# A fused attention, MLP and expert kernel: attention of batches 1 to 3 among the chunks of the first MLP, 32x32 transposes on VectorE, and state times w_in per batch in small TensorE tiles

## The chip, the cores and the metric

The kernel runs on one core of a Trainium2 chip. The metric is the device time of one execution in microseconds. A core has TensorE (PE in the profile), VectorE (DVE), ScalarE (ACT), GpSimd (POOL) and SyncE (SP), which here only issues DMAs. Each engine works through its own instructions in the order written, and they meet in semaphores. SBUF and PSUM have 128 partitions; PSUM has 8 banks of 512 float32 for each partition.

## The reference

Three layers follow each other. Everything is float32.

```
B, H, S, Ns, D = 4, 8, 512, 32, 64
scores = x @ state.T / sqrt(D);   xread = softmax(scores) @ state      # S rows of a batch
scores2 = state @ x.T / sqrt(D);  sread = softmax(scores2) @ x         # Ns rows of a batch
X = rows of all batches, heads side by side                            # (2176, 512)
h = X @ w_in;  g = h * tanh(log1p(exp(h)));  Y = g @ w_out             # 512 -> 2048 -> 512
logits = normalised(Y) @ normalised(expert_emb).T / tau                # 8 experts
out = softmax(logits)[best] * relu(Y @ w1[best]) @ w2[best]            # 512 -> 1024 -> 512
```

scores and scores2 are the same numbers, normalised once over the 32 states and once over the 512 positions.

## The kernel before

**Precision.** The large products run in the faster format float32r: each operand is split into a high and a low part, and a product is three matmuls (high by high, high by low, low by high). WH and WL hold the two parts of weights, Ah and Al those of the attention's probabilities, gh and gl those of the activation. Products that are not split run in float32; one such matmul leaves two MATMUL records and two LDWEIGHTS records in the trace.

**Attention.** xread is never formed. Since xread @ w_in = softmax(scores) @ (state @ w_in), the first MLP multiplies the probabilities with M = state @ w_in. `M(i)` makes M for all four batches at once: 128 columns (4 batches by 32 states) stand in the array, and for a pair of heads in the two halves of the partitions two matmuls of 64 rows work on two banks (line 487). ScalarE copies M to Mst (line 799), SyncE stores it to the DRAM scratch `state_w_in` (line 300), and it comes back per batch later and is split into WH and WL.

For each batch b, TensorE turns x in 16 transposes of 128x128 (`turn`, line 458), forms the scores in four float32 matmuls of 512 columns (`score`, line 468), and turns the scores, the exponentials E2 and the probabilities P1 (lines 479, 519, 529). sread is 16 float32 matmuls of 64 columns with 128 weight columns (line 536). VectorE and ScalarE take maxima, exponentials, sums and reciprocals between them. All four batches are done before `H(0)`: the loop over b starts batch b+1's turning and scores inside batch b.

**First MLP.** There are 4 chunks (one a batch, 512 rows each) of 8 units, and a unit is 256 of the 2048 hidden columns. `H(u)` is 12 matmuls of 512 columns (line 555) into banks 0 and 1, `Y(u)` 24 of them (line 581) into banks 2 to 5. Between them stands the activation of a unit: on ScalarE a tanh, two squares, two exponentials and the copy to gh, on VectorE five operations of 128x1024 (`mish_q`, `mish_e`, `mish_r`, `mish_g`, `mish_lo`). TensorE's order is written out: H runs two units ahead of Y, and H(u) waits for `mish_q` of unit u-1, which empties banks 0 and 1. Each chunk c above 0 also carries the routing of the chunk before it (`route_t` turns a tile of Y, `route_l` makes its logits, `route_k` ranks, and `route_a` and `route_b` are the VectorE part).

**The rows of sread.** The 128 rows of all batches (named z) go through two units of 1024 hidden columns with unsplit weights (line 565), placed in chunk 3; `GT` turns their activation and `YB` multiplies it with w_out.

**The end of the MLP.** After the last Y come the first expert tile (`PA`, `TR`, `PB`) and the routing of z and of chunk 3; then VectorE builds the table of tiles (lines 1372 to 1435). Only with the table does ScalarE load the second expert tile (line 913), and the loop over the expert tiles begins.

## Time and profile before

| | |
|---|---|
| time, median of 3 runs | 750.76 us (748.86 to 751.18) |
| profiled execution | 747.9 us, of which its span 746.1 us |
| PE, DVE, ACT busy | 90%, 57%, 55% of the span |
| first H(0) | 104.8 us |
| first Y of chunks 0, 1, 2, 3 | 120.6, 195.35, 268.96, 342.64 us |
| last Y ends | 445.45 us |
| second expert tile begins | 482.43 us |

The profile is one execution. Its span goes from the first to the last instruction. The chain of waits is followed back from the last instruction to what released each step. A matmul record's time overlaps the next record's, so costs of a group are read from when the group begins and when the next piece of the chain begins.

### The profile page before, as it was taken

How to read it: one execution, taken by the hardware profiler on the slowest of the kernel's cores; microseconds unless marked ns; L12 is line 12 of the kernel's file. 1: busy time of each engine (PE TensorE's matmuls, PEld its weight loads, DVE VectorE, ACT ScalarE, POOL GpSimd, SP SyncE). 2: the span in 40 equal slices, each digit the busy share in tenths (PEclk: the TensorE clock that was granted, in tenths of full speed). 3: DMA queues.
4: the chain of work that ended last, by engine and by line, in shares of the span. 5: the costliest groups of instructions: out<-in, count | busy, mean ns of one | idle time of the engine just before them, and what ended most of it. 6: DMA issues, size and time to landing. Idle time of an engine off the chain costs nothing.

```text
span 746.1 us, 10419 instructions
## 1 busy us (share of the span) xinstructions
PE 670.1 (90%) x3124; PEld 527.8 (71%) x3125; DVE 424.4 (57%) x629; ACT 408.3 (55%) x517; POOL 51.1 (7%) x73
## 2 busy tenths in 40 slices
PE   4778767999899999999989799199999999999995
PEld 3355456888688878887766688177888888888884
DVE  1456558888758876887476654553361262154261
ACT  1334578878887887789664735052352262243260
POOL 2000000000001100200011001200000000000001
PEclk9999997999999999999999899599999999999999
DMA  9575595211001210121304210374270162145140
GB/s 207 129 188 168 172 294 184 84 58 56 29 1 58 84 29 1 71 72 57 112 16 155 71 56 16 119 240 138 71 239 29 43 207 92 42 126 184 43 156 4
DMA packets 51150, 76.52 MB, mean 103 GB/s; under 512 B 21507, under 2 KB 21507, under 8 KB 51120
## 3 DMA queue, kind: packets, MB, share of 16 engines
q1 hardware_dynamic: 44912, 61.14, 26.8%
q0 software_dynamic: 3040, 9.13, 3.2%
q10 hardware_dynamic: 3168, 5.86, 2.7%
q8 instruction: 17, 0.28, 0.2%
q14 instruction: 13, 0.11, 0.0%
HBM read 56.47 MB, written 20.55 MB: 103 GB/s over the span
## 4 chain that ended last, share of the span: by engine, by line
PE 67%; ACT 17%; DVE 8%; issue 6%; DMA 1%; SPq 0%; ACTq 0%; POOL 0%; DVEq 0%; POOLq 0%
PE PS L661 16%; PE PS L683 16%; PE PS L581 12%; PE PS L555 6%; ACT rr L854 3%; ACT WH L780 3%; ACT ww L844 3%; DVE ww L1156 2%; PE PS L468 2%; ACT gh L865 2%; ACT rr L852 2%; PE PS L670 2%; PE PS L565 2%; PE PS L536 2%; PE PS L624 2%
## 5 line engine op out<-in xcount | busy, mean ns | idle before, releaser
L581 PE MATMUL PS<-WH,gh 128*128 128x512 f32 x256 | 103.1, 403 | 4.7 <-DVE ysb L1188 4.7
L581 PE MATMUL PS<-WL,gh 128*128 128x512 f32 x256 | 101.6, 397 | 0.0
L581 PE MATMUL PS<-WH,gl 128*128 128x512 f32 x256 | 101.5, 397 | 0.0
L1246 DVE TENSOR_TENSOR WL<-raw,WH 128x1024 f32 (+1 forms) x48 | 56.8, 1221 | 31.8 <-ACT WH L917 31.8
L683 PE MATMUL PS<-WH,hh 128*128 (+1 forms) x168 | 68.5, 407 | 2.3 <-DVE hl L1256 2.3
L1151 DVE SCALAR_TENSOR_TENSOR qq<-ww,PS 128x1024 f32<-128x1024 f32 x34 | 41.5, 1220 | 44.2 <-ACT ww L846 43.9
L683 PE MATMUL PS<-WL,hh 128*128 (+1 forms) x168 | 66.0, 393 | 0.0
L683 PE MATMUL PS<-WH,hl 128*128 (+1 forms) x168 | 65.9, 393 | 0.0
L935 ACT ACTIVATE hh<-PS 128x512 fp32r<-128x512 f32 x42 | 22.8, 595 | 78.6 <-PE PS L670 76.6
L917 ACT ACTIVATE WH<-raw 128x1024 f32 (+1 forms) x48 | 48.5, 1056 | 31.1 <-issue 22.9
L858 ACT ACTIVATE ww<-ww,cst 128x1024 f32<-128x1024 f32 x34 | 39.2, 1153 | 39.8 <-DVE ww L1156 39.8
L581 PEld LDWEIGHTS PS<-WH,gh 128*128 128x128 f32 x256 | 48.8, 191 | 16.7 <-issue 5.9
L1156 DVE SCALAR_TENSOR_TENSOR ww<-ww,rr 128x1024 f32<-128x1024 f32 x34 | 41.7, 1225 | 27.9 <-ACT rr L854 27.9
L581 PEld LDWEIGHTS PS<-WH,gl 128*128 128x128 f32 x256 | 48.6, 190 | 11.6
L581 PEld LDWEIGHTS PS<-WL,gh 128*128 128x128 f32 x256 | 48.9, 191 | 11.0
L1251 DVE TENSOR_TENSOR yl<-PS,yh 128x512 fp32r<-128x512 f32 x21 | 14.5, 692 | 71.0 <-ACT yh L923 71.0
L661 PE MATMUL PS<-WH,yh 128*128 (+1 forms) x168 | 48.7, 412 | 4.5 <-issue 2.7
L929 ACT ACTIVATE hsb<-PS 128x512 f32<-128x512 f32 x42 | 24.5, 595 | 50.2 <-PE PS L661 48.9
L555 PE MATMUL PS<-Ah,WH 128*128 128x512 f32 x128 | 42.5, 414 | 8.2 <-DVE qq L1151 8.2
L844 ACT ACTIVATE ww<-PS 128x1024 f32<-128x1024 f32 x34 | 34.5, 1016 | 26.8 <-PE PS L555 17.9
L661 PE MATMUL PS<-WL,yh 128*128 (+1 forms) x168 | 46.7, 401 | 0.0
L661 PE MATMUL PS<-WH,yl 128*128 (+1 forms) x168 | 46.7, 401 | 0.0
(220 smaller groups left out, 1255.0 us busy)
## 6 DMA issues: line engine op xcount, KB each, us to landing
raw<-in_w SPq DMA_DIRECT2D x48, 512.0 KB, 4.2
raw<-in_w_in SPq DMA_DIRECT2D x16, 512.0 KB, 5.0
state_w_in<-Mst SPq DMA_DIRECT2D x64, 128.0 KB, 2.3
raw<-state_w_in SPq DMA_DIRECT2D x16, 512.0 KB, 3.6
yg<-by_expert ACTq DMA_DIRECT2D x22, 260.0 KB, 2.7
xb<-in_x SPq DMA_DIRECT2D x16, 256.0 KB, 5.6
raw<-in_w_out SPq DMA_DIRECT2D x8, 512.0 KB, 4.6
by_expert<-junk SPq DMA_DIRECT2D x1, 2080.0 KB, 10.3
```

What stands on the lines that cost most here:

```text
L555: mm = pe.matmul(PS[:, e, :], w[:, p // 2, o:o + P], a[:, c, g, :], start=(i == 0 and g == 0), stop=(i == 2 and g == HG - 1))
L581: mm = pe.matmul(PS[:, 2 + t, :], a[:, v % 2, e, t * P:t * P + P], w[:, 8 + p, e * 512:e * 512 + 512], start=(p == 0 and e == 0 and i == 0 ...
L661: mm = pe.matmul(PS[:, j, :], a[:, k, :], w[:, bass.ds(slot + k, 1), j * 512:j * 512 + 512].rearrange("p o n -> p (o n)"), start=(i == 0 a ...
L683: mm = pe.matmul(PS[:, 5, :], a[:, m, :], w[:, bass.ds(slot + (KT + m // 2), 1), (m % 2) * 512:(m % 2) * 512 + 512].rearrange("p o n -> p ...
L844: a.activation(ww[:, u % 2], PS[:, 0:2, :], ACT.Tanh, scale=0.5).then_inc(t_rdy, 1)
L858: a.activation(ww[:, u % 2], ww[:, u % 2], ACT.Square, bias=cst[:, 0:1]).then_inc(s_rdy, 1)
L917: a.activation(WH[:, bass.ds(slot + b, 1), :].rearrange("p o n -> p (o n)"), raw[:, b % NSTAGE], ACT.Copy).then_inc(w_hi, 1)
L929: a.activation(hsb[:, j * 512:j * 512 + 512], PS[:, j, :], ACT.Relu).then_inc(hs_rdy, 1)
L935: a.activation(hh[:, 4 * j:4 * j + 4, :], PS[:, 3 + j, :].rearrange("p (k m) -> p k m", k=4), ACT.Copy).then_inc(hh_rdy, 1)
L1151: v.scalar_tensor_tensor(out=qq[:, u % 2], in0=ww[:, u % 2], scalar=4.0, in1=PS[:, 0:2, :], op0=ALU.subtract, op1=ALU.mult).then_inc(q_rdy, 1)
L1156: v.scalar_tensor_tensor(out=ww[:, u % 2], in0=ww[:, u % 2], scalar=4.0, in1=rr[:], op0=ALU.add, op1=ALU.mult).then_inc(e_rdy, 1)
L1246: v.tensor_tensor(WL[:, bass.ds(slot + b, 1), :].rearrange("p o n -> p (o n)"), raw[:, b % NSTAGE], WH[:, bass.ds(slot + b, 1), :].rearran ...
```

## The change

Only batch 0's attention stands ahead of the first MLP. Batch c+1's stands inside chunk c: `score` after Y of unit 0, `M(c+1, 0..2)` before Y of units 5 to 7, `sread` after Y of unit 5, `sread_turned` after unit 6, `M(c+1, 3)` after unit 7. The VectorE part is dealt over the eight units (`turn_x`, `soft_1` to `soft_5`, `A_lo`, `sread_scale`), as is the ScalarE part.

TensorE's transposes of x, the scores, E2 and P1 are gone. VectorE transposes blocks of 32x32 instead. For that x lies in SBUF in another layout (X2, 16 DMAs a batch where there were 4), and the state is laid out block by block (S2, st32, stBD). sread is now 128 matmuls a batch, each on 32 partitions with 32 weight columns and 64 moving columns; the four j of a step use four different 32x32 tiles of the array and write four different groups of partitions of the same bank.

M is made per batch: 8 matmuls of 512 columns, each on 64 partitions with 32 weight columns, into four groups of 32 partitions of two banks. It is split from PSUM into WH and WL straight away (`M_hi`, `M_lo`), so the scratch, its 64 stores and 16 loads are gone, and w_in is read from DRAM once for each batch. M(c+1, 0) waits for `A_lo(c+1)`.

The units of z move to after units 2 and 3 of chunk 3, with matmuls into banks 6 and 7. At the end chunk 3 is routed before z, and `YB(2)`'s second half and `YB(3)` stand behind the last Y.

```diff
     SEQ = [("m", c, p) for c in range(B) for p in range(PC)]
-    SEQ.insert(3 * PC + 4, ("z", B, 0))
-    SEQ.insert(3 * PC + 7, ("z", B, 1))
+    SEQ.insert(3 * PC + 3, ("z", B, 0))
+    SEQ.insert(3 * PC + 5, ("z", B, 1))
...
+    STREAM = []
+    for what in ([(0, 0), 0, (0, 1), 1, (0, 2), 2, 3, (0, 3), 4, 5, 6, 7]
+                 + [(c, nb) for c in range(1, B) for nb in range(NB)] + ["z0", "z1", "z2", "z3"]):
+        if isinstance(what, int):
+            STREAM.append(("o", what))
+        elif isinstance(what, str):
+            STREAM += [("z", int(what[1]), 0), ("z", int(what[1]), 1)]
+        else:
+            STREAM += [("w", NB * what[0] + what[1], 0), ("w", NB * what[0] + what[1], 1)]
...
             def load_x(b):
-                for t in range(ST):
-                    sp.dma_start(xb[b][:, t].rearrange("p (h d) -> p h d", h=H),
-                                 x[b].rearrange("h (p t) d -> t p h d", t=ST)[t]).then_inc(in_x[b], 16)
...
+                if b >= 2:
+                    sp.wait_ge(sr_mm, b - 1)
+                for u in range(2):
+                    for j in range(4):
+                        for g in range(HG):
+                            sp.dma_start(X2[b % 2][u][32 * j:32 * j + 32, :, D * g:D * g + D], x_v[b, j, u, g]).then_inc(in_x[b], 16)
...
+                if r >= NSTAGE:
+                    kind, k, *_ = STREAM[r - NSTAGE]
+                    sp.wait_ge({"w": m_mm, "o": o_lo, "z": hz_mm}[kind], k + 1)
+                kind, k, *g = STREAM[r]
+                src = w_out_v[k] if kind == "o" else w_in_v[k % NB, g[0]]
...
+                pe.wait_ge(x_tr, 4 * b + 4)
+                if b > 0:
+                    pe.wait_ge(m_lo, NB * b)
                 for g in range(HG):
...
+            def M(c, nb, bank=6):
+                k = NB * c + nb
+                if k > 1:
+                    pe.wait_ge(m_lo, k - 1 if c == 0 else k)
+                if c == 0 and nb == 3:
+                    pe.wait_ge(sh_e, 2)
+                if nb == 0 and c > 0:
+                    pe.wait_ge(idx_rdy, c - 1)
+                    pe.wait_ge(a_lo, c + 1)
+                if nb == 1 and c > 0:
+                    pe.wait_ge(shn_rdy, 2 * c + 2)
+                if nb == 2 and c > 0:
+                    pe.wait_ge(sh_e, 2 * c + 2)
+                for g in range(HG):
+                    r = RING["w", k, g]
+                    pe.wait_ge(in_w[r % NSTAGE], 16 * (r // NSTAGE + 1))
+                    for kk in range(2):
+                        for h in range(2):
+                            j = 32 * (2 * kk + h)
+                            mm = pe.matmul(PS[j:j + 32, bank + g, :], stA[64 * h:64 * h + 64, 2 * g + kk, NS * c:NS * c + NS],
+                                           raw_v[64 * h:64 * h + 64, r % NSTAGE, kk, :], start=True, stop=True)
+                mm.then_inc(m_mm, 1)
...
+            def sread(b):
+                pe.wait_ge(e2d_rdy, b + 1)
+                if b > 0:
+                    pe.wait_ge(m_lo, NB * b + 1)
+                for g in range(HG):
+                    for t in range(16):
+                        for j in range(4):
+                            mm = pe.matmul(PS[32 * j:32 * j + 32, 6, D * g:D * g + D], E2D[32 * j:32 * j + 32, g, 32 * t:32 * t + 32],
+                                           X2[b % 2][t // 8][32 * j:32 * j + 32, t % 8, D * g:D * g + D],
+                                           start=(t == 0), stop=(t == 15))
+                mm.then_inc(sr_mm, 1)
+
+            def sread_turned(b):
+                pe.wait_ge(shn_rdy, 2 * b + 2)
+                if b > 0:
+                    pe.wait_ge(m_lo, NB * b + 2)
+                for g in range(HG):
+                    mm = pe.transpose(PS[0:D, 7, g * P:g * P + P], shn[:, g, :], ident[:])
+                mm.then_inc(sh_t, 1)
...
+            for v in range(B * PC):
+                c, p = v // PC, v % PC
+                if v + 2 < B * PC:
+                    H(v + 2)
...
+                if c < 3 and p >= 5:
+                    M(c + 1, p - 5)
...
+                if c < 3:
+                    if p == 0:
+                        if c == 0:
+                            M(0, 3)
+                        score(c + 1)
+                    if p == 5:
+                        sread(c + 1)
+                    if p == 6:
+                        sread_turned(c + 1)
+                    if p == 7:
+                        M(c + 1, 3)
...
+            for t in range(ST):
+                route_t(3, t)
+            for t in range(ST):
+                route_l(3, t)
+            YB(2, (2, 3))
+            YB(3, (0, 1))
+            route_k(3)
+            YB(3, (2, 3))
...
+            def M_hi(c, nb, bank=6):
+                k = NB * c + nb
                 act.wait_ge(m_mm, k + 1)
-                if k >= 4:
-                    act.wait_ge(m_out[k % 4], 64 * (k // 4))
...
+            def M_lo(c, nb, bank=6):
+                k = NB * c + nb
+                dve.wait_ge(m_hi, k + 1)
+                v.tensor_tensor(WL[:, k % NM].rearrange("p (g n) -> p g n", g=HG), PS[:, bank:bank + 2, :],
+                                WH[:, k % NM].rearrange("p (g n) -> p g n", g=HG).bitcast(F32), ALU.subtract).then_inc(m_lo, 1)
...
+            def turn_x(b, c):
+                dve.wait_ge(in_x[b], 256)
+                if b > 0:
+                    dve.wait_ge(sr_mm, b)
+                for u in range(2):
+                    ins = v.transpose(xT[:, c, u * 256:u * 256 + 256].rearrange("p (t n) -> p t n", n=32),
+                                      X2[b % 2][u][:, :, 32 * c:32 * c + 32])
+                ins.then_inc(x_tr, 1)
...
+            def soft_1(b):
+                dve.wait_ge(sc_e, b + 1)
+                v.transpose(PT[:], SC[:]).then_inc(av, 1)
+                dve.wait_ge(av, AV * b + 1)
+                v.tensor_reduce(r1[:, 0, :], pv, AX, ALU.max).then_inc(av, 1)
+                dve.wait_ge(av, AV * b + 2)
+                v.tensor_tensor(pv, pv, r1[:, 0, :].unsqueeze(2).to_broadcast(wide), ALU.subtract).then_inc(p1_d, 1)
...
+            def soft_4(b):
+                dve.wait_ge(pn_rdy, b + 1)
+                dve.wait_ge(s2_x, 2 * b + 2)
+                v.transpose(SC[:], PT[:]).then_inc(af_rdy, 1)
+
+            def soft_5(b):
+                dve.wait_ge(s2_x, 2 * b + 2)
+                v.tensor_scalar(r2[:, 2, :], r2[:, 2, :], 1e-9, None, ALU.add).then_inc(bv, 1)
+                dve.wait_ge(bv, 2 * b + 1)
+                v.reciprocal(r2[:, 3, :], r2[:, 2, :]).then_inc(bv, 1)
+                v.transpose(E2D[:], E2[:]).then_inc(e2d_rdy, 1)
+
+            def A_lo(b):
+                dve.wait_ge(a_hi, b + 1)
+                v.tensor_tensor(Al[:, b % 2], SC[:], Ah[:, b % 2].bitcast(F32), ALU.subtract).then_inc(a_lo, 1)
...
+                    if n == 0:
+                        turn_x(c + 1, 0)
+                        turn_x(c + 1, 1)
+                    if n == 1:
+                        turn_x(c + 1, 2)
+                        turn_x(c + 1, 3)
+                    if n == 3:
+                        soft_1(c + 1)
+                    if n == 4:
+                        soft_3(c + 1)
+                    if n == 5:
+                        soft_4(c + 1)
+                    if n == 6:
+                        A_lo(c + 1)
+                        soft_5(c + 1)
+                    if n == 7:
```

TensorE, from its first matmul on. Before (SN is the state, xb x, E and P the exponentials and probabilities):

```order
L458 MATMUL PS<-ident,xb_92 128x128 x16
L495 MATMUL PS<-ident,SN_85 128x128 x4
L468 MATMUL PS<-ysb,stT 128x512 x4
L501 MATMUL PS<-ident,E_90 128x8 x4
L479 MATMUL PS<-ident,SC 128x128 x8
L458 MATMUL PS<-ident,xb_93 128x128 x16
L468 MATMUL PS<-ysb,stT 128x512 x4
L487 MATMUL PS<-raw,stA 128x512 x4
L519 MATMUL PS<-ident,E_90 128x128 x8
L487 MATMUL PS<-raw,stA 128x512 x4
L529 MATMUL PS<-ident,P_89 128x128 x8
L536 MATMUL PS<-E_90,xb_92 128x64 x16
```

After (x_0a and x_0b are the halves of X2, E2D the turned exponentials, shn the scaled sread, WH and Ah the operands of H(0)):

```order
L494 MATMUL PS<-ident,SN_91 128x128 x4
L444 MATMUL PS<-xT,stBD 128x512 x4
L467 MATMUL PS<-raw,stA 32x512 x8
L502 MATMUL PS<-ident,en 128x8 x4
L467 MATMUL PS<-raw,stA 32x512 x8
L478 MATMUL PS<-x_0a,E2D 32x64 x32
L478 MATMUL PS<-x_0b,E2D 32x64 x32
L478 MATMUL PS<-x_0a,E2D 32x64 x32
L478 MATMUL PS<-x_0b,E2D 32x64 x32
L467 MATMUL PS<-raw,stA 32x512 x8
L488 MATMUL PS<-ident,shn 64x128 x2
L526 MATMUL PS<-Ah,WH 128x512 x2
```

Of the attention that was repeated for each batch, one batch is left ahead of the first row that reads Ah; the rows of 8 and 16 transposes are gone (three small ones are left, of the state, the expert embedding and shn), and sread has become 4 rows of 32.

VectorE, unit 6 of chunk 0 with the row ahead of it. Before (WL<-raw is the rest of a weight block):

```order
L1065 TENSOR_TENSOR WL<-raw,WH 128x1024
L1151 SCALAR_TENSOR_TENSOR qq<-ww,PS 128x1024
L1174 TENSOR_TENSOR gl<-qq,gh 128x1024
L1156 SCALAR_TENSOR_TENSOR ww<-ww,rr 128x1024
L1161 SCALAR_TENSOR_TENSOR qq<-qq,rr 128x1024
L1168 SCALAR_TENSOR_TENSOR qq<-ww,qq 128x1024
L1065 TENSOR_TENSOR WL<-raw,WH 128x1024
```

After, from the end of unit 5 on (E_53 is E2, r_68 its sums, Al<-SC is `A_lo(1)`):

```order
L1202 SCALAR_TENSOR_TENSOR qq<-ww,qq 128x1024
L1090 TENSOR_TENSOR WL<-raw,WH 128x1024
L1131 STREAM_TRANSPOSE SC<-PT 128x1024
L1185 SCALAR_TENSOR_TENSOR qq<-ww,PS 128x1024
L1208 TENSOR_TENSOR gl<-qq,gh 128x1024
L1190 SCALAR_TENSOR_TENSOR ww<-ww,rr 128x1024
L1195 SCALAR_TENSOR_TENSOR qq<-qq,rr 128x1024
L1202 SCALAR_TENSOR_TENSOR qq<-ww,qq 128x1024
L1142 TENSOR_TENSOR Al<-SC,Ah 128x1024
L1135 TENSOR_SCALAR r_68<-r_68 128x2
L1137 RECIPROCAL r_68<-r_68 128x2
L1138 STREAM_TRANSPOSE E2D<-E_53 128x1024
```

`soft_4` now follows unit 5, and `A_lo(1)` and `soft_5` unit 6; in TensorE's order M(1, 0), which waits for `A_lo(1)`, stands between H(7) and Y(5).

## Rows read from the trace of the kernel before

**Rows 1.** The page: span, busy time of the engines, the chain by engine.

```profile
span 746.1 us, 10419 instructions
PE 670.1 (90%) x3124; PEld 527.8 (71%) x3125; DVE 424.4 (57%) x629; ACT 408.3 (55%) x517; POOL 51.1 (7%) x73
...
PE 67%; ACT 17%; DVE 8%; issue 6%; DMA 1%; SPq 0%; ACTq 0%; POOL 0%; DVEq 0%; POOLq 0%
```

**Rows 2.** Stretches: length, each engine's busy us, TensorE clock, DMA share, GB/s.

```profile
0.00:104.80 104.80, 76.37 (x393) 48.17 (x394) 49.42 (x82) 43.44 (x72) 5.15 (x25) 0.97 0.70 181
104.80:120.60 15.80, 7.60 (x27) 5.47 (x26) 11.87 (x11) 14.12 (x16) 0.00 (x0) 0.85 0.86 316
120.60:195.35 74.75, 72.26 (x300) 58.22 (x301) 62.53 (x55) 63.08 (x63) 0.00 (x0) 0.96 0.21 72
195.35:268.96 73.61, 72.50 (x340) 59.70 (x341) 56.65 (x71) 59.31 (x67) 6.57 (x10) 1.00 0.13 44
...
342.64:445.45 102.81, 94.94 (x405) 72.49 (x406) 63.65 (x90) 63.49 (x74) 7.31 (x6) 0.95 0.24 80
445.45:482.43 36.98, 21.22 (x128) 17.71 (x128) 19.30 (x93) 11.45 (x23) 6.13 (x6) 0.80 0.14 48
```

**Rows 3.** The chain of waits, ahead of H(0): start, us, what.

```profile
14.52 6.57 PE PS L468 x8
...
44.48 0.88 PE PS L479 x8
...
66.18 0.88 PE PS L479 x8
```

**Rows 4.** The chain of waits in the first MLP and at its end.

```profile
201.60 2.74 PE PS L555 x12
204.34 0.79 PE PS L624 x8
205.62 5.58 PE PS L581 x24
...
359.79 6.87 PE PS L565 x16
...
389.44 8.58 PE PS L565 x16
...
404.05 2.72 PE PS L601 x12
...
467.58 0.17 DVE idx L1242
...
475.41 0.18 DVE tab L1435
```

**Rows 5.** SyncE in order of time: start, us, operation.

```profile
0.78 2.96 SPq L288 DMA_DIRECT2D xb<-in_x  x4
...
3.78 2.63 SPq L325 DMA_DIRECT2D SN<-in_state  x4
```

**Rows 6.** Groups of instructions up to 104.8 us: shapes, count | busy, mean ns | idle before.

```profile
L1071 DVE COPY ysb<-PS 128x512 f32<-128x512 f32 x8 | 5.5, 687 | 16.8 <-PE PS L458 16.8
L1136 DVE TENSOR_TENSOR P<-P,lg 128x1024 f32<-128x1024 f32 x4 | 4.9, 1224 | 0.1
...
L799 ACT ACTIVATE Mst<-PS 128x1024 f32<-128x1024 f32 x16 | 16.4, 1028 | 25.8 <-PE PS L487 25.7
```

**Rows 7.** TensorE's small products in order of time: start, us, engine, operation.

```profile
21.02 0.33 PEld L501 LDWEIGHTS PS<-ident,E 8*128 8x128 f32 x4 [0.89 <-issue]
27.44 3.67 PE L468 MATMUL PS<-ysb,stT 128*128 128x512 f32 x8 [1.12 <-ACT ysb L786]
31.04 1.13 PE L487 MATMUL PS<-raw,stA 64*128 64x512 f32 x4
40.73 3.76 PE L536 MATMUL PS<-E,xb 128*128 128x64 f32 x32
```

More of the change, by code:

```diff
@@ new lines, in H, with HB @@
+                mm.then_inc(h_mm, 1)
+            def HB(p):
+                pe.wait_ge(sh_e, 2 * B)
+                pe.wait_ge(m_lo, NB * B)
+                if p == 1:
+                    pe.wait_ge(q_rdy, Z0 + 1)
+                for e in range(2):
+                    for g in range(HG):
+                        r = RING["z", 2 * p + e, g]
+                        pe.wait_ge(in_w[r % NSTAGE], 16 * (r // NSTAGE + 1))
+                        for j in range(2):
+                            mm = pe.matmul(PS[:, 6 + e, :], sh[:, 2 * g + j, :], raw_v[:, r % NSTAGE, j, :],
+                                           start=(g == 0 and j == 0), stop=(g == 1 and j == 1))
+                    mm.then_inc(hz_mm, 1)
@@ new lines, in _ @@
+                if kind == "m" and c < 3:
+                    if n == 2:
+                        scores_out(c + 1)
+                    if n == 4:
+                        exp_2(c + 1)
+                if kind == "m" and c > 0 and n == 0:
+                    sread_out(c)
+            mish_hi(LAST)
+            load(t0)
+            whi(0, 0, 0)
+            whi(0, 1, 0)
+            split_gz(2)
+            whi(0, 2, 0)
+            split_gz(3)
+            y_hi(t0)
+            whi(0, 3, 0)
@@ new lines, in _ @@
+            pn_rdy, bv = sem("pn_rdy"), sem("bv")
+            dve.wait_ge(in_state, 192)
+            v.transpose(st32[:].rearrange("p b c n -> p (b c n)"), S2[:].rearrange("p b g d -> p (b g d)")).then_inc(st_32, 1)
+            dve.wait_ge(st_zero, 1)
+            dve.wait_ge(st_32, 1)
+            for j in range(4):
+                v.tensor_copy(stBD[32 * j:32 * j + 32, :, :, 32 * j:32 * j + 32], st32[32 * j:32 * j + 32]).then_inc(st_d, 1)
+            for c in range(2 * HG):
+                turn_x(0, c)
@@ L1142, in _ @@
-            split_lo(("m", 0, 0))
-            split_lo(("o", 0))
-            split_lo(("m", 0, 1))
-            split_lo(("o", 1))
+            v.tensor_scalar(en[:], eb[:], es[:, 2:3], None, ALU.mult).then_inc(en_rdy, 1)
+            soft_1(0)
+            soft_2(0)
+            M_lo(0, 0, 2)
+            soft_3(0)
+            soft_4(0)
+            soft_5(0)
+            dve.wait_ge(en_t, 1)
+            v.tensor_copy(enT[:], PS[:, 1, 0:KT * E].rearrange("p (k e) -> p k e", k=KT)).then_inc(enT_rdy, 1)
@@ L1149, in mish_q @@
+            A_lo(0)
+            o_rest(0)
+            M_lo(0, 1, 4)
+            sread_scale(0)
+            M_lo(0, 2, 2)
+            o_rest(1)
             def mish_q(u):
+                bank = 0 if SEQ[u][0] == "m" else 6
                 dve.wait_ge(w_rdy, u + 1)
-                v.scalar_tensor_tensor(out=qq[:, u % 2], in0=ww[:, u % 2], scalar=4.0, in1=PS[:, 0:2, :],
+                v.scalar_tensor_tensor(out=qq[:, u % 2], in0=ww[:, u % 2], scalar=4.0, in1=PS[:, bank:bank + 2, :],
                                        op0=ALU.subtract, op1=ALU.mult).then_inc(q_rdy, 1)
@@ L1312, in _ @@
                     mish_lo(u - 1)
-                if u == Z0 + 2:
-                    lo_gz(0)
-                if u == Z0 + 3:
-                    lo_gz(1)
-                if u == LAST:
-                    lo_gz(2)
+                if kind == "m" and n < 3 and c > 0:
+                    M_lo(c, n + 1)
+                if n == 7 and c < 3:
+                    M_lo(c + 1, 0)
+                if n == 4 and c < 3:
+                    soft_2(c + 1)
+                if done >= 0 and n == (6 if c == 3 else 5):
+                    route_a(done)
@@ L1355, in _ @@
+                if c == 3 and n == 6:
+                    lo_gz(0)
+                if c == 3 and n == 7:
+                    first_expert()
+                    lo_gz(1)
+            mish_lo(LAST)
+            wlo(0, 0, 0)
+            wlo(0, 1, 0)
+            lo_gz(2)
+            wlo(0, 2, 0)
+            lo_gz(3)
+            y_lo(t0)
+            wlo(0, 3, 0)
+            y_out(3)
+            turned(3, 1)
+            turned(3, 3)
+            route_a(3)
+            route_b(3)
             y_out("z")
@@ L1363, in _ @@
             route_b("z")
-            wlo(0, 7, 0)
-            route_a(3)
-            route_b(3)
             def wide(ap):
```

807 lines of the change are left out of this document (329 added, 478 removed).

## The prediction

> **What bounds the kernel now.** I read the page first. TensorE is busy for 90% of the span and makes 67% of the chain that ended last, so the question of every edit is what it does to TensorE's work and to its idle time [rows 1]. Then I cut the execution at the first H(0), at the first Y of each chunk and at the second expert tile [rows 2]. The reader is to see three kinds of stretch there. Up to H(0) TensorE is busy for 76.4 of 104.8 us. In chunk 1 it is busy for 72.5 of 73.6 us, while DVE has 57 and ACT 59: TensorE alone sets this pace, and every microsecond put on it comes out at the end. At the end of the MLP (445.45 to 482.43) it is busy for 21 of 37 us, and what counts is the chain of routing and table. The chain of waits says what a batch costs ahead of H(0): the same row stands at 44.48 and at 66.18, so a batch takes 21.7 us [rows 3].
>
> So the change takes three batches out of a stretch in which TensorE was idle for a quarter, and puts them into one in which it was idle for 1.5%. The gain must come from the new form costing TensorE less than 21.7 us a batch. I sum on TensorE.
>
> **The prices of the new work on TensorE.** score(b) has the same shape: 3.67 us [rows 7], I take 3.7.
>
> M: two float32 matmuls of 64 rows on the two halves of the partitions take 1.13 us, four records (line 487), where eight records of the full height take 3.67, 0.43 of 512 columns each beside the last one's end [rows 7]. Alone four would take 1.7, so different halves of the rows do run together. A call of M now has 8 matmuls on four small tiles, in two rounds. If the quarters of the columns run together as the halves of the rows do, it is 2 x 1.08 = 2.2 us, at least 2.0. If only the rows do, 4 x 0.86 + 0.3 = 3.7. If nothing does, 8 x 0.86 = 6.9. I take 2.2, since the trace shows side by side work of tiles, and 14 calls are on TensorE's path: M(0,2) ahead of H(0), M(0,3), and 12 more.
>
> sread: 128 matmuls or 256 records of 64 columns a batch, where 32 records took 3.76 us, 0.117 each [rows 7]. Bounds: if the four tiles run together, one tile has 64 records at 0.43 x 64/512 = 0.054 us, 3.5 us. At the old spacing it is 256 x 0.112 = 28.7. The closest small records are four weight loads in 0.33 us of about 0.14 each, 0.064 apart (line 501), 16.4 us. Those four load 128 columns and the new ones 32, so it should be less. I take 10 us, half way between 3.5 and 16.4.
>
> The rows bound this only widely. The Trainium skill (TensorE: Matmul & The Clock Gate, "Wait — 56ns, not 53.3ns?") states a floor of about 25 ns from start to start of small matmuls, and 62 ns where the instructions are decoded in microcode. By the one an sread is 6.4 us (estimate, 256 x 25 ns) and the sum falls by 4 x 3.6 = 14 us; by the other it is 15.9 and the sum rises by 24. No row here is short enough to tell them apart.
>
> **Ahead of H(0).** Only batch 0 is left, but its loads come later. x is now 16 DMAs, then 8 of S2 and 4 of SN2. Four loads of SN took 2.63 us and four of xb 2.96 [rows 5], so 28 issues of 0.6 us would end at 18 us; with some at 0.45 and 3 us to land I take 18 for the last state. Before, TensorE began its scores at 14.5 [rows 3]. Then in one chain: on DVE st32 0.7, four copies 1.8, eight `turn_x` 2.3 (a 128x512 copy is 0.69 [rows 6]; I price a 32x32 transpose as a copy of its size); score(0) 6.6, as the first one took before at the low clock [rows 3]; scores to SBUF 1.1; `soft_1` 3.65, three operations of 128x1024 at 1.22 [rows 6]; `soft_2` 1.4; M_lo 1.2, which stands in between; `soft_3` 3.1; `soft_4` 1.2; `soft_5` 1.6; sread(0) 10; M(0,2) and the turn of sread 2.5. This gives 55.3 us for H(0), against 104.8: 49.5 us less. The start of the pipeline up to Y(0), 15.8 us with TensorE half idle [rows 2], stays.
>
> **Inside chunks 0 to 2.** Each gets 3.7 (score) + 10 (sread) + 4 x 2.2 (M) + 0.3 = 22.8 us of TensorE, and chunk 0 also M(0,3), 2.2: 70.6 us in all. That the scratch with its 64 stores and 16 loads goes saves nothing here, since no step of the chain in the MLP waits for it; the DMAs move 44 GB/s in chunk 1 [rows 2], and w_in read three times more (12 MB over some 290 us) adds 41.
>
> DVE gets 14.8 us a batch more: three transposes of 1024 and four of 512, four passes over the probabilities, one reduction, `A_lo`. 56.7 + 14.8 = 71.5 stands beside 73.6 + 22.8 = 96 of TensorE, so DVE isn't the bound of a chunk. But it is late at one place. M(c+1,0) waits for `A_lo(c+1)`, which is queued behind all of unit 6, and unit 6 behind `soft_1` to `soft_4`, which make units 3 and 4 about 10 us of DVE each where TensorE's slots are 9. Laying the units one after the other with rows of 1.22 on DVE and 1.03 on ACT [rows 6], `A_lo` ends 2.6 us after H(7), with Y(5) queued behind M: 2.6 x 3 = 7.8 us.
>
> The small tiles are light work. The second unit of z took 8.58 us where the first took 6.87 [rows 4], since the clock had fallen to the low level for a while: 1.7 us each time. I put this down once a chunk, 5.1 us. With 0 and 13 as its ends this and the wait are in the range.
>
> **Chunk 3 and the end.** Unchanged in amount: units of 2.74 + 5.58 us and some more, z's units 6.87, YB 2.72, a tile's logits 0.79 [rows 4]. It has 94.2 us of TensorE, of which the halves of YB that now stand behind the last Y (5.5 us) are no part; with 3 us of waits 97, where it took 102.8 [rows 2]. Behind the last Y the new chain is: copy out, four turns and logits, `route_a` (8.2 us), YB and rank and `route_b` (12.3), then z, whose expert work is in between (24.7), the table 7.7 (32.4; before, from 467.7 to 475.4 [rows 4]), load and turn of the next tile 7.0 (39.4; before, from 475.4 to 482.4). That is 39.4 where 37.0 were. Both together: 3 us less. It could be 8 less or 3 more.
>
> **Sum.** -49.5 + 70.6 + 7.8 + 5.1 - 3 = +31 us. The profiled execution has 746.1 of span in 747.9 of time and lies 0.4% under the median of the runs, 750.76. I add to the median: 782 us.
>
> **Rivals.**
> 1. *The small tiles run side by side almost fully.* For it: the 1.13 us of line 487. Against: nothing shows that records can be issued every 20 ns. With sread 5 and M 2.0: -54.7 + 53 + 7.8 - 3 = +3, 754 us.
> 2. *Issue or the column quarters bind.* For it: the 0.064 of line 501. sread 16.4 alone gives +57 and M 3.7 alone +52, so about 805 us; both 828.
> 3. *Tiles that write the same bank take turns.* Before, the two row halves of line 487 wrote two banks (6 and 7); now two halves, and in sread four quarters, write one bank. So the row's overlap was only seen with separate banks. M would be 6.9 and sread 28.7: -26 + 188 + 10 = +172, 922 us. The Trainium skill (TensorEngine Tiling (Array Packing), "Gotcha 1: PSUM Pressure") says just this, that different row tiles cannot access the same PSUM bank at the same time. The tiles here also write different partitions, which the rule doesn't speak of, and I give it 3 in 100.
> 4. *The prologue's gain outweighs the rest.* One mechanism: sread at its tile limit. It decides in four places, one ahead of H(0) and three in the chunks, and the sum is -52.7 + 4 x sread + 14 x M + waits and clock. With M 2.2 and 7.8 of waits it crosses zero at sread = 3.5 us. At sread 3.5, M 2.0 and 3 us of waits it is -7.7: 743 us, faster.
> 5. *DVE's transposes cost twice a copy.* Nothing in the trace shows one. Then H(0) is 6.3 us later and each chunk waits some 3 us more: 797 us.
>
> **How the numbers follow.** Forecast 0.45 (own range 765 to 800), rival 1 0.20, rival 2 0.15, rival 3 0.03, rival 4 0.12, rival 5 0.05. The likeliest time is 782. For 8 in 10 the range runs from 746 to 815: it leaves out about half of rival 4, rival 3 and the end of rival 2. Within 0.3% (2.3 us, about what can be told from no change) lies a part of rival 1, 0.04; faster is rival 4 and a little of rival 1, 0.14; slower 0.82.
>
> **What would show it.** H(0) at 55 us, with the last state DMA at 18. An L478 group of 128 matmuls 10 us long, an L467 group of 8 about 2.2. Chunks 1 and 2 some 100 us long instead of 73.6, with TensorE busy above 95%. A wait of L467 for `A_lo` (L1142) of 2 to 3 us, three times. 39 us from the last Y to the second expert tile. I am wrong if sread is under 5 or above 16 us, if M is above 3, or if TensorE waits for DVE for more than 8 us in a chunk.

## The result

The changed kernel takes 766.22 us (median of 4 runs, 763.33 to 770.77); the kernel before, run beside it, 749.81 us (745.24 to 751.18). The ratio is 1.0235, 95% interval 1.0167 to 1.0303: slower. The profiled execution took 765.84 us, of which 763.7 is the span, against 747.9 and 746.1 before.

### The profile page after: what moved, and what is told of

Its sections match the earlier page's. It is cut to its first block, busy times and chain, and to the rows that moved or that the text cites. A ratio compares the mean times of both kernels' runs of the same rounds, so it can differ in the third digit from the quotient of the medians.

```text
span 763.7 us, 12248 instructions
## 1 busy us (share of the span) xinstructions
PE 672.9 (88%) x4060; PEld 513.7 (67%) x4061; DVE 438.4 (57%) x656; ACT 385.7 (51%) x483; POOL 53.2 (7%) x73
## 4 chain that ended last, share of the span: by engine, by line
PE 58%; DVE 18%; issue 12%; ACT 7%; DMA 3%; SPq 2%; ACTq 0%; POOL 0%; DVEq 0%; POOLq 0%
PE PS L649 15%; PE PS L671 14%; PE PS L555 8%; PE PS L526 6%; PE PS L467 3%; PE PS L444 3%; DVE ww L1190 2%; PE PS L658 2%; ACT ww L870 2%; DVE qq L1202 2%; DVE qq L1185 2%; PE PS L478 2%; DVE gl L1208 1%; DMA raw<-in_w 1%; PE PS L630 1%
## 5 line engine op out<-in xcount | busy, mean ns | idle before, releaser
L555 PE MATMUL PS<-WH,gh 128*128 128x512 f32 x256 | 104.1, 407 | 0.0
L555 PE MATMUL PS<-WL,gh 128*128 128x512 f32 x256 | 101.6, 397 | 0.0
L555 PE MATMUL PS<-WH,gl 128*128 128x512 f32 x256 | 101.4, 396 | 0.0
L1185 DVE SCALAR_TENSOR_TENSOR qq<-ww,PS 128x1024 f32<-128x1024 f32 x34 | 41.2, 1211 | 65.5 <-ACT ww L858 65.5
L671 PE MATMUL PS<-WH,hh 128*128 (+1 forms) x168 | 68.7, 409 | 4.8 <-DVE hl L1294 4.8
L671 PE MATMUL PS<-WH,hl 128*128 (+1 forms) x168 | 66.9, 398 | 0.0
L671 PE MATMUL PS<-WL,hh 128*128 (+1 forms) x168 | 66.6, 397 | 0.0
L555 PEld LDWEIGHTS PS<-WH,gh 128*128 128x128 f32 x256 | 48.9, 191 | 18.8 <-issue 8.3
L555 PEld LDWEIGHTS PS<-WH,gl 128*128 128x128 f32 x256 | 48.6, 190 | 11.5
L555 PEld LDWEIGHTS PS<-WL,gh 128*128 128x128 f32 x256 | 48.9, 191 | 10.6
L526 PE MATMUL PS<-Ah,WH 128*128 128x512 f32 x128 | 45.7, 439 | 11.1 <-DVE qq L1185 11.1
L1190 DVE SCALAR_TENSOR_TENSOR ww<-ww,rr 128x1024 f32<-128x1024 f32 x34 | 41.6, 1224 | 18.7 <-ACT rr L866 18.7
```

Source lines behind the costliest of these rows:

```text
L526: mm = pe.matmul(PS[:, e, :], w[:, (NB * c + p // 2) % NM, o:o + P], a[:, c % 2, g, :], start=(i == 0 and g == 0), stop=(i == 2 and g == H ...
L555: mm = pe.matmul(PS[:, 2 + t, :], a[:, v % 2, e, t * P:t * P + P], w[:, 8 + p, e * 512:e * 512 + 512], start=(p == 0 and e == 0 and i == 0 ...
L671: mm = pe.matmul(PS[:, 5, :], a[:, m, :], w[:, bass.ds(slot + (KT + m // 2), 1), (m % 2) * 512:(m % 2) * 512 + 512].rearrange("p o n -> p ...
L1185: v.scalar_tensor_tensor(out=qq[:, u % 2], in0=ww[:, u % 2], scalar=4.0, in1=PS[:, bank:bank + 2, :], op0=ALU.subtract, op1=ALU.mult).then ...
L1190: v.scalar_tensor_tensor(out=ww[:, u % 2], in0=ww[:, u % 2], scalar=4.0, in1=rr[:], op0=ALU.add, op1=ALU.mult).then_inc(e_rdy, 1)
```

## The profile after

The page of the changed kernel, which answers to [rows 1]. TensorE is busy for about as long as before (672.9 us for 670.1), and the span is 17.6 us longer: what was added is mostly idle time of TensorE and time at the low clock.

```profile
span 763.7 us, 12248 instructions
PE 672.9 (88%) x4060; PEld 513.7 (67%) x4061; DVE 438.4 (57%) x656; ACT 385.7 (51%) x483; POOL 53.2 (7%) x73
...
PE 58%; DVE 18%; issue 12%; ACT 7%; DMA 3%; SPq 2%; ACTq 0%; POOL 0%; DVEq 0%; POOLq 0%
```

The stretches of the changed kernel, columns as in [rows 2], cut at H(0), H(2), the first Y of chunks 1, 2 and 3, the end of the last Y and the second expert tile:

```profile
0.00:50.20 50.20, 19.86 (x322) 9.77 (x324) 21.45 (x37) 10.05 (x16) 5.13 (x25) 0.90 0.44 129
50.20:65.00 14.80, 7.60 (x26) 5.48 (x24) 10.79 (x13) 12.35 (x14) 0.00 (x0) 0.86 0.76 197
65.00:172.66 107.66, 95.71 (x646) 67.84 (x647) 78.73 (x83) 66.87 (x70) 0.00 (x0) 0.92 0.39 108
172.66:267.49 94.83, 90.24 (x672) 67.04 (x670) 70.96 (x95) 64.10 (x75) 7.09 (x9) 0.98 0.17 57
267.49:360.78 93.29, 88.67 (x671) 66.36 (x670) 68.31 (x87) 64.14 (x75) 6.21 (x5) 1.00 0.18 57
360.78:455.09 94.31, 88.38 (x382) 66.59 (x381) 60.49 (x86) 61.49 (x70) 5.54 (x6) 0.98 0.25 89
455.09:499.88 44.79, 29.98 (x154) 24.44 (x152) 23.23 (x98) 13.24 (x26) 8.82 (x7) 0.82 0.12 40
```

One correction to the text ahead: what it calls the first Y of chunk 0, at 120.6 us, is H(2); Y(0) stands some 5 us behind it. The stretch is cut at H(2) in both kernels here, so the comparison holds.

| stretch | before | after | difference | forecast |
|---|---|---|---|---|
| to H(0) | 104.8 | 50.2 | -54.6 | -49.5 |
| to H(2) | 15.8 | 14.8 | -1.0 | 0 |
| chunk 0 | 74.75 | 107.66 | +32.9 | +29.3 |
| chunk 1 | 73.61 | 94.83 | +21.2 | +27.1 |
| chunk 2 | 73.68 | 93.29 | +19.6 | +27.1 |
| chunk 3 | 102.81 | 94.31 | -8.5 | -5.8 |
| end, to the second tile | 36.98 | 44.79 | +7.8 | +2.4 |
| experts | 263.67 | 263.82 | +0.2 | 0 |
| sum | 746.1 | 763.7 | +17.6 | +31 |

What TensorE waited for in the changed kernel (engine, line, releaser: us in total, times, longest):

```profile
PE PS L526 <- DVE qq L1185: 11.1, 4, 3.7
...
PE PS L467 <- DVE Al L1142: 9.0, 3, 3.0
PE PS L478 <- DVE E2D L1138: 5.2, 1, 5.2
...
PE PS L467 <- DMA raw<-in_w_in: 4.7, 3, 2.8
...
PE PS L444 <- DVE WL L1085: 4.2, 3, 3.7
PE PS L478 <- issue: 4.1, 3, 1.4
```

The two disputed prices, from the chain of waits of the changed kernel, around Y(5) of chunk 0 (L555) (start, us, what):

```profile
133.76 1.92 PE PS L467 x16
135.68 5.78 PE PS L555 x24
141.46 3.69 PE PS L478 x250
145.15 1.36 issue
146.51 0.31 PE PS L478 x6
146.82 2.96 PE PS L526 x12
```

A call of M is 8 float32 matmuls in 16 records and takes 1.9 us. An sread is 256 records in 3.7 us of work, 14 ns from start to start, and a gap of 1.4 us that no semaphore explains: 5.2 us together, where I had put 10. The gap stands behind record 250 in chunk 0, 212 in chunk 1 and 174 in chunk 2. TensorE's rows behind the first two, in order of time (x6 and x44 are the records left, in brackets the idle time ahead and what ended it):

```profile
146.51 0.31 PE L478 MATMUL PS<-x_1b,E2D 32*32 32x64 f32 x6 [1.36 <-issue]
240.80 0.86 PE L478 MATMUL PS<-x_0b,E2D 32*32 32x64 f32 x44 [1.35 <-issue]
```

Ahead of H(0), chain of the changed kernel. The last load of state lands at 16.03, and once sread is done, TensorE still waits for a block of w_in that SP, held by the ring of four buffers, could only ask for at 43.07. sread(0), from 40.84 to 46.09, isn't on the chain that ends at H(0); VectorE's work on a block of w_out (L1090), SP's request and the load run past it, and TensorE waits 1.05 and 0.84 us for w_in in M(0, 2):

```profile
21.52 6.22 PE PS L444 x8
...
41.82 1.23 DVE WL L1090
43.07 0.37 SPq L312
...
43.48 5.53 DMA raw<-in_w_in
...
49.05 1.06 PE PS L467 x8
```

In chunk 0, score(1) stands behind Y(0) and M(0, 3) and waits for the first `M_lo(0, 3)` (L1085), which on DVE is queued behind all of unit 1; the granted clock over it is 0.54, so mostly at its low level (1.2 GHz), and it takes 6.73 us and not the 3.67 of chunk 1. H(3) follows, and the mish units after it:

```profile
80.64 1.14 DVE WL L1085
81.79 0.14 issue
81.92 6.73 PE PS L444 x8
88.65 2.79 PE PS L526 x12
```

At the end, z's last ranking (L622, L623) stands behind PB (L671), the second product of the first expert tile. Chain of the changed kernel:

```profile
474.96 0.80 PE PS L614 x8
...
478.24 1.21 DVE hl L1294 x2
479.49 4.57 PE PS L671 x12
484.06 0.16 PE PS L622 x2
```

The logits of z were there at 475.76. Some 1.4 us of small VectorE operations lie between logits and ranking (so in a version below), so the table waits for a ranking that could have run some 7 us earlier. The kernel before ranks z ahead of PB: it is the change that moved it behind PB's first half.

## The experiments

Intervals are of the ratio to the kernel before, which was run beside each of three groups of versions: 752.02 us beside the first four below, 751.14 beside the next four, 750.61 beside the last three.

### The changed kernel again

> The changed kernel as it is, beside the others of this call, so that they can be compared on one chip. The theory that adds up the stretches of its profile (prologue -54.6, start of the pipeline -1.0, chunks 0 to 2 +32.9, +21.2, +19.6, chunk 3 -8.5, the end +7.8 us) expects 17 to 18 us over the kernel before, a ratio of 1.023. If that profile was a lucky or unlucky execution, the ratio will lie outside 1.017 to 1.030.

766.22 us, ratio 1.0212 (1.0169 to 1.0255), span 762.5. It is the base of the three below.

### M(c+1, 0) without its wait for A_lo

```diff
-                    pe.wait_ge(a_lo, c + 1)
+                    pe.wait_ge(sc_e, c + 1)
```

> M(c+1, 0) waits for the copy of the scores (sc_e) in place of A_lo(c+1); both leave banks 6 and 7 free. Theory: the three waits of M for A_lo, 3.0 us each in the profile, are on TensorE's path with nothing to take their place, so the time falls by 9 us against the changed kernel (758 us where it has 767) and no wait of 1 us or more takes the place of L467's. Rival: VectorE is late as a whole, so the wait comes back behind M (at sread for E2D, or at H for q_rdy): the time falls by less than 3 us.

756.39 us, ratio 1.0048 (1.0022 to 1.0075): 9.8 us less than the base. The row L467 <- L1142 is gone, and no row of M and DVE takes its place. Chunks 0, 1 and 2, counted from their first Y here and below, take 98.5, 90.5 and 90.3 us, where the base has 101.8, 94.5 and 92.9. So the wait cost what it showed, three times 3 us, and was needed by nothing in M: what M reads and writes is free once the scores are copied out.

### z's ranking ahead of the expert tile's product

```diff
-            PB(t0, (0, 1, 2, 3))
             route_k("z")
-            PB(t0, (4, 5, 6, 7))
+            PB(t0)
```

with `gate_exp("z")` and `route_b("z")` moved up in ACT's and DVE's order.

> Behind the last Y the ranking of z (route_k, gate_exp, route_b) stands ahead of the first tile's second product and of its low parts, which come after it. In the profile z's logits end at 475.8 and the table begins at 485.2 us, with 2.4 us of low parts and 4.6 of PB on the chain between. Theory: the chain of routing and table sets the second tile's begin, so 5 to 7 us are saved. Rival: PB and the weights of the first expert set it, since they now end later: less than 2 us saved.

761.09 us, ratio 1.012 (1.0084 to 1.0155): 5.1 us less than the base. The first load of the expert loop lies 34.9 us behind the last Y (490.50, the last Y ends at 455.63), where it lay 39.3 behind it; in the kernel before it is 31.4. Chain of this version; the ranking now follows the logits at once, and PB comes after it:

```profile
475.50 0.81 PE PS L614 x8
...
477.69 0.39 PE PS L622 x2
...
490.50 2.75 DMA yg<-by_expert
```

### score(1) one unit later

```diff
-                        score(c + 1)
+                        else:
+                            score(c + 1)
+                    if p == 1 and c == 0:
+                        score(1)
```

with ACT's `scores_out(1)` in unit 3 instead of 2.

> In chunk 0 alone, score(1) stands behind Y(1) and not behind Y(0), and its copy to SBUF in unit 3 and not 2. In the profile score(1) waits 3.7 us for M_lo(0,3), which VectorE does at the end of unit 2, and then runs at the low clock (6.7 us where 3.7 is usual). Theory: wait and low clock both go, 4 to 8 us saved. Rival: the start of the pipeline in chunk 0 is bound by ScalarE and VectorE, so TensorE idles elsewhere instead: under 2 us saved.

759.97 us, ratio 1.011 (1.0071 to 1.015): 6.3 us less. The waits for L1088 (L1085 in the changed kernel) fall from 4.2 us to 0.5. At L467 1.2 us come back, where the waits for A_lo grow from 9.0 to 10.2, and at H the waits for L1185 fall from 11.1 to 8.9. The changed kernel from Y(0) on, and this version from its Y(0) on, in stretches (the granted clock is the number behind the last bracket):

```profile
70.30:80.00 9.70, 7.92 (x41) 5.03 (x39) 8.82 (x12) 8.11 (x8) 0.00 (x0) 0.96 0.22 63
80.00:91.30 11.30, 9.38 (x21) 5.04 (x22) 1.78 (x2) 1.06 (x2) 0.00 (x0) 0.70 1.05 319
```

```profile
69.00:79.30 10.30, 10.30 (x53) 7.02 (x52) 9.42 (x12) 8.15 (x8) 0.00 (x0) 1.00 0.31 90
79.30:91.00 11.70, 11.70 (x45) 8.28 (x44) 9.49 (x9) 8.27 (x8) 0.00 (x0) 1.00 1.13 306
```

Without the wait the granted clock stays at 1.00, and with it the 3.1 us that score(1) took longer at the low clock are saved too.

### All three together

The three edits above in one kernel.

> The changed kernel with the three edits of the first runs together: M(c+1, 0) waits for the softmax copies and not for A_lo, score(1) of chunk 0 after Y(1), and the ranking of z ahead of the tile's PB. Theory 1: the three waits lie in different places and are gone each for itself, so the gains of 9.8, 5.1 and 6.3 us add up: 766.2 - 21.2 = 745, some 7 us under the kernel before. Theory 2: they share something (TensorE gets to the same DVE queue earlier, and the clock or the next wait takes back what one of them gave): only the largest and part of the others, 752 to 757, no faster than before. In the trace, under theory 1: chunk 0 at 101, chunks 1 and 2 at 90 each, the stretch from the last Y to the second tile at 40 us.

741.1 us (738.99 to 744.74), ratio 0.9894 (0.9853 to 0.9936). The gains add up: 25.1 us under the base where the three alone are 21.2, and the 3.9 us between lie within the intervals of the versions. Chunks 0 to 2 take 88.6, 90.0 and 90.1; for chunk 0 that is well under the 101 that was expected. Its stretch of chunk 0:

```profile
69.60:158.26 88.66, 85.08 (x635) 61.05 (x634) 74.26 (x80) 63.08 (x66) 0.00 (x0) 1.00 0.47 130
```

TensorE is busy for 85.1 of 88.7 us, and the clock is 1.00 from Y(0) to the first Y of chunk 1, where the changed kernel has 0.95 over the same stretch (0.92 if it is cut at H(2)), the version without the wait for A_lo 0.94 and the one with the later score 0.96. One place where the edits help each other is in the trace: with the later score alone, M(1, 0) waits 4.2 us for A_lo and then takes 3.6 us at a granted clock of 0.50, not 1.9; without that wait both go. That a gain beyond the sum is the clock fits these rows, but it was not tried by itself.

### Half of the matmuls of sread

```diff
-                        for j in range(4):
+                        for j in (range(4) if b == 0 else range(2)):
```

> sread of batches 1 to 3 makes only the tiles of rows and columns 0 to 63 (j = 0, 1 of 0 to 3), half of its matmuls: 128 records in place of 256; the sums of the other half are left out. Theory 1, a limit of issue (each small matmul with its weight load costs 14 ns whatever tile it is in): 128 records in 1.8 us where 256 take 3.6. Theory 2, a limit of each tile (a 32x32 tile takes its next matmul after some 57 ns, and four tiles run side by side): the records then come 28 ns apart and the group stays at 3.6 us. The gap of 1.36 us put down to issue goes under theory 1 of the queue (the queue of fetched instructions runs empty after some 250 small ones) and stays if it belongs to what follows the group.

Chain of this version:

```profile
140.76 3.69 PE PS L478 x128
```

128 records take the 3.69 us of 256. So the 14 ns are no cost of an instruction. The 32x32 tile takes its next matmul after 55 ns (3.48 us from the first start to the last, in 63 steps), and four tiles run side by side. Each tile here has a quarter of the columns to itself, so whether the 55 ns belong to the tile or to its quarter isn't separated. The gap of 1.4 us, however, is gone. A single run took 765.04 us. In the bounds that I drew, 3.5 us was the right one for the work, and its reckoning, 64 records at 0.054 in each tile, was the mechanism.

### sread with all four tiles on the same rows

```diff
-E2D[32 * j:32 * j + 32, g, 32 * t:32 * t + 32], X2[b % 2][t // 8][32 * j:32 * j + 32, ...
+E2D[0:32, g, 32 * t:32 * t + 32], X2[b % 2][t // 8][0:32, ...
```

> sread with all four j on the same 32 rows (operands of partitions 0 to 31 for each j), still four groups of 32 columns; its sums are then other ones. Theory 1: it takes different row groups for matmuls to run side by side, tiles in one row group take turns: 57 ns apart, 256 of them 14.6 us in place of 3.6, and some 11 us more per chunk. Theory 2: different column groups are enough: the time stays 3.6 us.

```profile
146.64 3.69 PE PS L478 x250
150.33 1.06 issue
151.39 0.43 PE PS L478 x6
151.81 5.42 PE PS L526 x12
```

Still 3.69 us: tiles in different quarters of the columns run side by side also where they read the same rows. What differs comes behind it: H takes 5.42 us in place of 2.96, as the granted clock is at 0.50 from 152 to 157 us, and it was at 1.00 there in the changed kernel. This light work on a quarter of the rows was followed by a lower clock in each of the three chunks (0.66 in the five us behind it in the other two). A single run took 767.14 us.

### M on one half of the rows

```diff
-stA[64 * h:64 * h + 64, ...], raw_v[64 * h:64 * h + 64, ...]
+stA[0:64, ...], raw_v[0:64, ...]
```

> The products M with both h on the rows 0 to 63, where the changed kernel gives h = 1 the rows 64 to 127; four groups of 32 columns as before; its sums are then other ones. A call has 16 matmuls of 256 columns, 1.9 us. Theory 1: matmuls in one row group take turns, so each pair now shares the rows and the call takes all 16 one behind the other: 16 x 107 ns at full clock = 1.7 us for the four if they run at most four wide and 16 x 107 = 1.7 us is the sum of all, which by the measured 1.9 us per call would say that M never ran side by side at all; then the call stays at 1.9 us. Theory 2: M did run four wide (16 of 256 columns in the time of 4 to 5 of them would be 0.5 us): it did not, so the length of 1.9 us must be a limit of the column groups or of issue, and again nothing moves. Only if the two row halves ran side by side, each two wide, does the call grow, to 3.7 us.

The expectation was written on a wrong shape. M's 16 records are of 512 columns in float32, two for each of 8 matmuls, about 0.43 us each beside the last one's end; one behind the other they would take 6.9 us, and in the changed kernel they take 1.9, so four do run side by side. Here, too, a call takes 1.85 us:

```profile
153.84 1.85 PE PS L467 x16
```

None of my expected 3.7 us: the four quarters of the columns are enough, and the halves of the rows add nothing here, since the two j of each h already stand in their own column quarter. The single whole run (783.38 us) says nothing about M, as other values can give the experts another share of the rows. The last Y ends 9.2 us later than in the changed kernel; 4.7 of that are the three Y(5) behind the wait for A_lo, at a lower clock (8.28 us and not 5.78 in chunk 0, where the granted clock is 0.67), and the rest stays open.

### The loads ahead of H(0)

In one version, on top of the three edits: the 12 state loads issued by ACT, and the ring with w_in's third block ahead of w_out's first. To match, ACT's `o_split(0)` moves behind `M_hi(0, 1)`, and DVE's `o_rest(0)` behind `M_lo(0, 1)`.

```diff
-    for what in ([(0, 0), 0, (0, 1), 1, (0, 2), 2, 3, (0, 3), 4, 5, 6, 7]
+    for what in ([(0, 0), (0, 1), (0, 2), 0, 1, 2, 3, (0, 3), 4, 5, 6, 7]
-                    sp.dma_start(S2[...
+                    act.dma_start(S2[...
-                sp.dma_start(SN2[...
+                act.dma_start(SN2[...
```

> The version with the three edits (741.1 us) and two more, ahead of H(0) only: the 12 loads of state are issued by ACT beside SP's 16 of x, where SP issued all 28 one after the other (0.45 us each plus a gap of 0.04); and the ring of weights loads w_in's third block ahead of w_out's first, so that M(0,2) finds it. Theory 1: SP's issues and the DMA behind M(0,2) are both on the path to H(0). x then is issued by 8.6 us and landed by 11, 5 us earlier, and of the 3.7 us that TensorE waited for w_in ahead of M(0,2) 3 go: H(0) at 42 to 43 in place of 49.5, and 734 us. Theory 2: what the loads cost is the landing, not the issue: 28 transfers at once share the 16 DMA engines (0.55 busy in the first 20 us), the last one lands at 14 to 15 however they are issued, and H(0) moves by 3 us at most.

732.29 us (730.72 to 736.37), ratio 0.9767 (0.9716 to 0.9817). H(0) is at 41.6 us. ACT's issues are done at 6.2 and the last state lands at 9.3, where it was 16.0; the row L467 <- DMA raw is gone. Chain of this version:

```profile
6.18 3.14 DMA SN<-in_state
...
34.24 5.44 PE PS L472 x256
39.68 1.85 PE PS L461 x16
...
41.87 2.77 PE PS L520 x12
```

H(0) begins 7.9 us earlier than in the version with the three edits (49.5), and most of it is the issue: sread(0) begins at 34.24 and not at 40.17. The rest is sread itself, 5.4 us where it took 6.4, and M(0, 2) without its wait of 0.8 us, so that the order of the ring gave about 1 us. Of the 3.7 us of waits for w_in that the expectation counts ahead of M(0, 2), 2.9 stood in M(0, 1), where sread later waited 5.1 us for E2D, and were not on the path. So the row of 28 issues on one engine was on the path, not the transfer: theory 1. The Trainium skill (Trainium Kernel Development and Optimization, "Key Constraints") says that issuing from several engines concurrently only saves the sequencer's issue time; the trace agrees, and here that was 6.7 us at the landing.

### sread cut in two

```diff
+                    if e == 1 and mid is not None:
+                        sread(mid, (1,))
```

in H(8)'s loop over e, and only the first half of sread behind Y(5).

> The version with the three edits (741.1 us); sread of batches 1 to 3 is cut in two, 128 matmuls behind Y(5) and 128 between the two halves of H(8). Theory 1: the 1.1 to 1.5 us of idle time put down to issue comes from so many small matmuls and weight loads in a row (over 480 instructions in 5 us), and 128 of them ran without it; with 2.5 us of large matmuls in between it goes, three times, so 3 to 4 us less, if M(c+1,1), whose wait for DVE's sread_scale now has 2.4 us less cover, is not late. Theory 2: the gap is bound to the place in the program (a fetch that falls due there) and stays wherever the group is cut: no change, or some us more if M(c+1,1) waits.

739.27 us, ratio 0.9861 (0.9797 to 0.9924): 1.8 us under the version with the three edits, where 3 to 4 were expected, and less than the intervals can tell apart. The profile is clear: no row L478 <- issue is left, M(c+1, 1) isn't late, and chunks 0 to 2 take 88.1, 89.0 and 89.0 us where they took 88.6, 90.0 and 90.1.

```profile
128.56 1.99 PE PS L478 x128
130.55 1.58 PE PS L529 x6
132.14 2.00 PE PS L478 x128
134.14 1.59 PE PS L529 x6
```

With the half as many matmuls above, this bears out theory 1: without so many small instructions in a row there is no gap. But theory 2 is right about the place. The changed kernel and every version that leaves the group of 256 whole have the gap behind record 250 in chunk 0, 212 in chunk 1 and 174 in chunk 2, in all nine traces. So it is no matter of 250 in a row: it falls on a fixed place of the program, and shows only where enough small instructions come there in a row. That TensorE's instructions arrive too slowly at this place would fit both; no trace shows it.

### Both

> The two edits of the last runs together, on top of the three before. The loads act ahead of H(0), the cut of sread inside the chunks, so they add up if each is worth what it is said to: 7 us and 3 to 4 us, 730 us. If the cut brings a wait of M(c+1,1) for DVE, it is at or above the time of the version with the loads alone.

729.73 us (727.89 to 732.6), ratio 0.9727 (0.9678 to 0.9776), span 727.3: 2.7% under the kernel before. H(0) is at 41.6, chunks 0 to 2 take 88.2, 89.0 and 89.0 us. The stretch of its chunk 1:

```profile
149.90:238.90 89.00, 88.73 (x672) 66.23 (x671) 70.76 (x95) 64.00 (x75) 7.11 (x9) 1.00 0.18 60
```

There TensorE has no idle time left to give, and the 15.4 us over the 73.6 of the kernel before are about the prices of the new work: 3.7 for the score, 3.7 for sread, four times 1.9 for M and 0.3 for the turn, 15.3 together. It is the fastest of all; against the version with the loads alone the 2.6 us are again within the intervals.

## Why the prediction was right in its sign, and where it was off

The mechanism held: three batches moved out of a stretch where TensorE was idle for a quarter into one where it alone sets the pace, and came out there nearly in full. The forecast, 782, was 16 us too high: 13.4 in the sum of the table, the rest in the medians, which lie 16.4 us apart where the profiled spans lie 17.6 apart, and in the base, 750.76 for 749.81. That the error is no larger is in part luck: sread, M and the clock were priced too high by more than that, and waits and an end that I didn't foresee took much of it back. 766 lies at the low end of my own range for the forecast (765 to 800) and nearer to rival 1's 754 than to 782.

- **sread at 10 us was the term that was mis-sized.** It measured 5.2, 3.7 of work and 1.4 of gap. The work stood at the lower bound, 3.5; I took half way to 16.4, a figure from four loads of 128 columns that [rows 7] had, a row of another kind. Three times 4.8 in the chunks and some 3 ahead of H(0) (below) are 17 us, more than the whole error. The gap was in none of the rows I used; waits of the same kind do stand among the large matmuls of the experts in the kernel before (L661, put down to issue, 1.6 and 1.1 us).
- **M at 2.2 us** measured 1.9: 4 us over 14 calls. Its reckoning (quarters of the columns run together) is shown by its 16 records.
- **Ahead of H(0)** I forecast 55.3 (the terms listed add up to 55.15) and it was 50.2. Up to the start of sread the terms give 42.65 and it was 40.84, as the last state was there at 16.0 and not at 18. sread took 5.2, not 10. M(0, 2) and the turn of sread took 4.1, not 2.5, with 1.9 us of waiting for w_in, which I had not listed at all. So sread isn't what H(0) waited for. At 10 us it would have been: it would have ended at 50.8, and H(0) begun some 3 us later than it did (an estimate, with my 2.5 behind it). I counted SP's issues ahead of the state but not the ring of four buffers behind them.
- **The wait for A_lo** was forecast at 2.6 us three times; it is 3.0 three times, and taking it away gave 9.8 us. The term was right; laying out the units with the durations of [rows 6] was enough to see it.
- **The clock.** I put 1.7 us a chunk. In chunks 1 and 2 it is 0.98 and 1.00, so almost nothing; in chunk 0 it is 0.95 from Y(0) on. It came not from the small tiles, as I had argued, but together with the waits: without them the clock is 1.00 with the same small tiles in place. The row that I took it from had a wait, too: ahead of z's second unit in the kernel before TensorE was busy for 0.4 of 3.0 us (386 to 389), and granted 0.58 over the next 4.
- **Not foreseen:** score(1)'s wait for `M_lo(0, 3)`, 3.7 us and 3.1 more of low clock, in chunk 0; moving the score by one unit gave 6.3 us. I had looked for what DVE owes M, and not for what it owes the score. Two waits of H for `mish_q` (L1185) in chunk 0, 3.9 us in all, were not in the sum either; the one of 2.8 is gone in the version with the later score.
- **DVE's transposes** cost as copies: 1.24 us for 128x1024, where a copy-like operation has 1.22 [rows 6]. Rival 5 is refuted.
- **DMA.** I had 41 GB/s more in the chunks; chunks 1 and 2 have 57 where they had 44. I left out that the 16 loads of the scratch, 512 KB each, go. Nothing on the path rests on it.
- **Chunk 3 and the end** were forecast at -3 and are -0.7. The end grew by 7.8, not 2.4. z's ranking waited behind PB, which I had put down as work in between and not as something that could be moved; that is worth 5.1 us. The kernel before had it ahead of PB.

Of the rivals, the first was nearest: sread 5 and M 2.0, 754 us. Its prices are what was measured, and it fell short by 12 us because it had neither the clock, nor score(1)'s wait, nor the end. Rival 2 falls: with half of its matmuls sread takes as long, so issue is no limit, and in M and sread the column quarters run side by side. Rival 3 would have had M at 6.9 and sread at 28.7. The Trainium skill (TensorEngine Tiling (Array Packing), "Gotcha 1: PSUM Pressure") says that different row tiles cannot access the same PSUM bank at the same time. Here four 32x32 tiles on four row groups, writing 32 partitions each of one bank, take 3.69 us for 256 records, as do two of them for 128 and four on the same rows: no sign of taking turns. Its figure of about 25 ns from start to start (TensorE: Matmul & The Clock Gate, "Wait — 56ns, not 53.3ns?") isn't a floor for tiles side by side either, since 14 ns were measured; a single tile's 55 ns lies above it. Rival 4, faster, had M and the work of sread right, but not the gap (5.2 us where it had 3.5, four times) and the waits (9.0 for A_lo alone where it had 3): with three places of waiting out, the same work was 1.1% faster than the kernel before.

## What to carry to other kernels

Moving work into a stretch that one engine fills costs its full price there, so the price has to be less than what it took outside. It was: what made this change slower were some 21 us of order, in three places, each to be read from a row of the form "X waited for Y, so many times" together with what is queued ahead of Y on its own engine. Price small matmuls on separate tiles by one tile's row of matmuls, not by the number of instructions, and look for a load that a ring of buffers holds back, not only for loads that stand in a row.

## What was not expected of the hardware

- Four 32x32 tiles in four quarters of the columns run side by side even on the same 32 rows and into the same bank: 256 matmul records of 64 columns, each with its weight load, in 3.69 us.
- Within such a group of 256 at full clock TensorE pauses for 0.9 to 1.6 us, behind record 250, 212 or 174 according to the chunk and at the same record in the traces of all versions with an uncut group; not in a group of 128, and not where 6 large matmuls stand between two groups of 128. Batch 0's sread, which falls into a stretch of lower clock, has no gap and takes 5.0 us from its first start to its last.
- A wait of 3 to 4 us in the chunks can be followed by the low clock: score(1) took 6.73 us against 3.67. Work of the same kind on 32 rows only was followed by it as well (H 5.42 us against 2.96).
